# Value splits held back in the opening, four more products in the first expert's routing, token numbers as one sum: clustered attention and two expert layers on one core

## The reference, cut to what matters

```python
# attention, B=2, H=8, S=768, D=64, 16 clusters per head
q_assign = argmax(q_n @ c_n.T); k_assign = argmax(k_n @ c_n.T)     # normalised rows
scores = where(q_assign == k_assign, q @ k.T / 8, -1e9)
x = softmax(scores) @ v                                            # 1536 rows of 512
# first expert layer: 8 experts, each takes exactly 192 of the 1536 rows
for idx in argsort(-(x @ w_gate).flatten()):                       # the largest logit first
    tok, e = idx // 8, idx % 8
    if assigned[tok] >= 0 or counts[e] >= 192: continue
    assigned[tok] = e; counts[e] += 1
out[assigned == e] = relu(x[assigned == e] @ w1[e]) @ w2[e]        # 512 -> 1024 -> 512
# second layer: 4 experts, all rows through each, weighted by p
p = domain_probs / (domain_probs.sum(-1) + 1e-9)
out += p[:, e] * (relu(x @ w1[e]) @ w2[e])
```

## Time and profile before

| | |
|---|---|
| runs | 1019.85, 1019.0, 1020.62 us (median 1019.85) |
| profiled execution | 1019.42 us, span of its instructions 1017.6 us |
| mean granted TensorE clock | 0.995 |
| busy share of the span | TensorE 98%, VectorE 60%, ScalarE 44%, GpSimd 42% |
| opening, up to the first exponential | 20.4 us |
| routing with the first expert layer's products | about 297 to 515 us |

### The profile page before, as it was taken

The page is one execution under the profiler, slowest core; times in us unless marked ns, Lnnn a source line. Parts: engine busy times, 40 slices in busy tenths (PEclk is TensorE's granted clock), DMA queues, the critical chain, the costliest instruction groups (busy, mean ns, idle before and its releaser), DMA issues.

```text
span 1017.6 us, 18267 instructions
## 1 busy us (share of the span) xinstructions
PE 999.1 (98%) x6642; PEld 921.0 (91%) x6642; DVE 611.8 (60%) x1355; ACT 444.6 (44%) x862; POOL 425.4 (42%) x349
## 2 busy tenths in 40 slices
PE   8999999999999999999999999999999999999997
PEld 7889999999988999999999889999889998889995
DVE  6888888888867455556045445554486554455543
ACT  5888888888830111113342333322343323223320
POOL 5233233332201111112456757556567765566542
PEclk8999999999999999999999999999999999999999
DMA  5232323223155555556722122122112321221201
GB/s 159 56 78 67 86 73 85 77 81 82 31 126 182 183 182 181 182 182 205 249 75 83 42 83 72 53 84 67 57 63 83 125 83 45 80 83 51 74 1 63
DMA packets 87314, 99.63 MB, mean 98 GB/s; under 512 B 18097, under 2 KB 57041, under 8 KB 87249
## 3 DMA queue, kind: packets, MB, share of 16 engines
q1 hardware_dynamic: 84960, 92.38, 30.0%
q0 software_dynamic: 2288, 6.36, 1.9%
HBM read 79.81 MB, written 6.32 MB: 85 GB/s over the span
## 4 chain that ended last, share of the span: by engine, by line
PE 93%; DVE 3%; ACT 1%; POOL 1%; issue 1%; DMA 0%; DVEq 0%; POOLq 0%
PE ps_y L1569 10%; PE ps_y L1568 10%; PE ps_y L1567 10%; PE ps_h L1594 8%; PE ps_y L1609 8%; PE ps_h L1569 7%; PE ps_h L1567 7%; PE ps_h L1568 7%; PE ps_t L1448 6%; PE ps_s L1435 4%; PE ps_o L1462 3%; PE ps_o L1463 3%; PE ps_s L1436 3%; PE ps_m L1482 2%; PE ps_m L1409 2%; PE ps_m L1395 1%
## 5 line engine op out<-in xcount | busy, mean ns | idle before, releaser
L623 POOL TENSOR_TENSOR w_lo<-w_sum,w_hi 128x1792 fp32r<-128x1792 f32 x32 | 129.9, 4083 | 62.4 <-ACT w_hi L829 62.4
L1569 PE MATMUL ps_y<-b_lo,h_hi 128*128 128x512 f32 x384 | 149.7, 390 | 0.0
L1568 PE MATMUL ps_y<-b_hi,h_lo 128*128 128x512 f32 x384 | 149.7, 390 | 0.0
L1567 PE MATMUL ps_y<-b_hi,h_hi 128*128 128x512 f32 x384 | 149.4, 389 | 0.0
L1357 DVE SCALAR_TENSOR_TENSOR Y<-ps_y,ids_all,Y 128x512 f32<-128x512 f32 x84 | 63.0, 750 | 134.9 <-PE ps_y L1569 134.9
L1567 PE MATMUL ps_h<-x_hi,w_hi 128*128 128x384 f32 x384 | 128.6, 335 | 0.0
L1569 PE MATMUL ps_h<-x_lo,w_hi 128*128 128x384 f32 x384 | 128.5, 335 | 0.0
L1568 PE MATMUL ps_h<-x_hi,w_lo 128*128 128x384 f32 x384 | 128.4, 334 | 0.0
L629 POOL TENSOR_TENSOR b_lo<-b_raw,b_hi 128x2048 fp32r<-128x2048 f32 x16 | 74.0, 4622 | 116.2 <-ACT b_hi L836 115.4
L1008 DVE TENSOR_TENSOR p_lo<-ps_t,p_hi 128x384 fp32r<-128x384 f32 x192 | 99.9, 548 | 26.7 <-ACT p_hi L749 25.2
L999 DVE TENSOR_REDUCE neg_max<-ps_s 128x1 f32<-128x768 f32 x96 | 91.3, 951 | 14.8 <-PE ps_s L1436 14.3
(11 more groups left out here) (241 smaller groups left out, 2221.6 us busy)
## 6 DMA issues: line engine op xcount, KB each, us to landing
w_sum<-in_moe_w_dram SPq DMA_DIRECT2D x64, 256.0 KB, 3.2
b_raw<-in_moe_w_dram SPq DMA_DIRECT2D x16, 1024.0 KB, 5.2
raw_a<-in_moe_w_dram SPq DMA_DIRECT2D x8, 1024.0 KB
raw_b<-in_moe_w_dram SPq DMA_DIRECT2D x8, 1024.0 KB, 8.4
odd_a<-in_moe_w_dram SPq DMA_DIRECT2D x8, 1024.0 KB
odd_b<-in_moe_w_dram SPq DMA_DIRECT2D x8, 1024.0 KB, 8.3
khhT<-kqT SPq DMA_DIRECT2D x32, 192.0 KB, 3.1
raw_k<-in_k_dram SPq DMA_DIRECT2D x16, 192.0 KB, 2.4
```

The costliest lines, as they stand in the source:

```text
L623: g.tensor_tensor(w_lo[t][:], w_sum[t][:, 1:8], w_hi[t][:].bitcast(F32), ALU.subtract).then_inc(wlo_done[t], 1)
L1567: t_.matmul(dst, w_hi, x_hi, start=first, stop=False)
L1568: t_.matmul(dst, w_lo, x_hi, start=False, stop=False)
L1569: return t_.matmul(dst, w_hi, x_lo, start=False, stop=last)
```

## The change

- GpSimd waits for `one_ready >= 4`, the one-hots of the first two heads, before `split_first_values`. What follows on GpSimd is queued behind it.
- Eight more fillers (18 for 10) before the second head's cluster products.
- `F_FIRST` has two products for one behind the last three counts of phase 1, and six for five ahead of its ranks: four products more in phase 1, four fewer at the end of the list.
- The token number stands in three columns of `place` whose sum it is (4 times, 2 times, and the rest), and one reduction per number takes the place of copy and multiply-add. `place` is 15 columns wide and not 14.
- In phase 0 the closing of the chosen expert (three VectorE instructions) moves behind the first two token numbers.
- ScalarE copies `xe` in two halves, and TensorE's first product waits for the first half, the third for the second.

The places in the code that only shift columns are left out of the diff.

```diff
--- before.py
+++ after.py
@@ -52,7 +52,7 @@
     FAR = -(2.0 ** 100)
     BIG = 2.0 ** 125
 
-    F_FIRST = (0,) * 4 + (3, 1, 3, 1, 3, 1, 5, 0)
+    F_FIRST = (0,) * 4 + (3, 2, 3, 2, 3, 2, 6, 0)
     F_SECOND = (14, 2, 10, 2, 9, 2, 9, 2, 9, 2, 11, 0)
     F_PHASE = (12, 2, 7, 2, 6, 2, 6, 2, 6, 2, 9, 0)
     F_TOKENS = [0, 0, 8] + [8] * (E - 4)
...
@@ -96,8 +96,8 @@
         weigh = sb("weigh", [P, ND, P], BF16)
         first_e = sb("first_e", [P, E], F32)
         first_c = sb("first_c", [P, C], F32)
-        place = sb("place", [P, NT, 2 + 3 * E2], BF16)
-        place_f = sb("place_f", [P, NT, 2], F32)
+        place = sb("place", [P, NT, 3 + 3 * E2], BF16)
+        place_f = sb("place_f", [P, NT, 3], F32)
         rows = ExitStack()
         X = sb("X", [P, NT, H * (D + E)], F32, rows)
         rows.close()
...
@@ -199,7 +199,6 @@
         rank = sb("rank", [P, 2, NT], F32)
         slot = sb("slot", [P, 2, NT, 2], BF16)
         pen = sb("pen", [P, NT], F32)
-        place_lo = sb("place_lo", [P, 2], F32)
         ids = sb("ids", [P, E, 2, 1 + E2], I32)
         mix_lo = sb("mix_lo", [P, 2, E2], F32)
         mix_mid = sb("mix_mid", [P, 2, E2], F32)
...
@@ -501,11 +500,12 @@
                    allow_small_or_imprecise_dtypes=True).then_inc(const_ready, 1)
             g.iota(first_c[:], [[-1, C]], base=C, channel_multiplier=0,
                    allow_small_or_imprecise_dtypes=True).then_inc(const_ready, 1)
-            for i, (pattern, mult) in enumerate((([[P, B], [0, TPB]], 1), ([[0, B], [1, TPB]], 0))):
+            for i, (pattern, mult) in enumerate((([[4 * P, B], [0, TPB]], 4), ([[2 * P, B], [0, TPB]], 2),
+                                                   ([[0, B], [1, TPB]], 0))):
                 g.iota(place_f[:, :, i], pattern, base=0, channel_multiplier=mult,
                        allow_small_or_imprecise_dtypes=True).then_inc(const_ready, 1)
-            pool.wait_ge(const_ready, 9)
-            g.tensor_copy(place[:, :, 0:2], place_f[:]).then_inc(const_ready, 1)
+            pool.wait_ge(const_ready, 10)
+            g.tensor_copy(place[:, :, 0:3], place_f[:]).then_inc(const_ready, 1)
 
             def search_constants():
 
...
@@ -583,6 +583,7 @@
             pool.wait_ge(rows_split, 2)
             split_second(0, k_rows, qkv[1])
             split_second(1, q_rows, qkv[0])
+            pool.wait_ge(one_ready, 4)
             split_first_values()
             split_second_values()
             split_head(1, 0)
...
@@ -861,7 +862,8 @@
 
             def rows_1(m):
                 act.wait_ge(xt_full, m + 1)
-                s.copy(xe[:].rearrange("p (a c) m -> p a c m", a=2), xe_ps).then_inc(xe_done, 1)
+                for a in range(2):
+                    s.copy(xe[:, 2 * a:2 * a + 2, :], xe_ps[:, a]).then_inc(xe_done, 1)
 
             def y_out(m, j):
                 act.wait_ge(y_full, 2 * m + j + 1)
...
@@ -944,7 +946,7 @@
             clink(v_.reciprocal(cen_s[:, 6:7], cen_s[:, 5:6]))
             v_.tensor_scalar(cen2[:], spread(cen[:], 1, [P, 2, D]), cen_s[:, 6:7], None,
                              ALU.mult).then_inc(cen_rows, 1)
-            dve.wait_ge(const_ready, 10)
+            dve.wait_ge(const_ready, 11)
             dve.wait_ge(zeros_done, 2)
             dve.wait_ge(cen_hi, 1)
             v_.tensor_tensor(cenT[:, :, 1, :], ps_o[:, 0:P].rearrange("p (h c) -> p h c", c=C),
...
@@ -1146,39 +1148,37 @@
                     v_.tensor_tensor(rows_hot[:, :, c0:c1, :], spread(steps_2[:, c0:c1, :], 1, hot),
                                      spread(slot[:, n % 2], 2, hot), ALU.is_equal).then_inc(hot_ready, 1)
 
-            W = 2 + 3 * E2
+            W = 3 + 3 * E2
 
             def token_ids(n):
 
                 HS = CAP // 2
                 dve.wait_ge(ids_full, n + 2)
                 at = ps_tok[0:HS, 0:2 * W].rearrange("p (s a) -> p s a", s=2)
-                link(v_.tensor_copy(place_lo[0:HS, :], at[:, :, 1]))
-                v_.scalar_tensor_tensor(out=ids[0:HS, n, :, 0], in0=at[:, :, 0], scalar=float(TPB),
-                                        in1=place_lo[0:HS, :], op0=ALU.mult, op1=ALU.add).then_inc(ids_ready, 1)
+                with nc.allow_low_precision(reason="whole numbers under 2 ** 24"):
+                    v_.tensor_reduce(ids[0:HS, n, :, 0], at[:, :, 0:3], AX.X, ALU.add).then_inc(ids_ready, 1)
 
             def first_token_ids(s):
 
                 HS = CAP // 2
                 dve.wait_ge(ids_full, s + 1)
                 at = (ps_tok, ps_tok_0)[s]
-                link(v_.tensor_copy(place_lo[0:HS, s:s + 1], at[0:HS, 1:2]))
-                v_.scalar_tensor_tensor(out=ids[0:HS, 0, s, 0:1], in0=at[0:HS, 0:1], scalar=float(TPB),
-                                        in1=place_lo[0:HS, s:s + 1], op0=ALU.mult, op1=ALU.add).then_inc(ids_ready, 1)
+                with nc.allow_low_precision(reason="whole numbers under 2 ** 24"):
+                    v_.tensor_reduce(ids[0:HS, 0, s, 0:1], at[0:HS, 0:3], AX.X, ALU.add).then_inc(ids_ready, 1)
 
             def first_token_mix():
 
                 HS = CAP // 2
                 for s in range(2):
-                    add(v_.tensor_copy(mix_lo[0:HS, s], (ps_tok, ps_tok_0)[s][0:HS, 2 + 2 * E2:W]))
+                    add(v_.tensor_copy(mix_lo[0:HS, s], (ps_tok, ps_tok_0)[s][0:HS, 3 + 2 * E2:W]))
                 dve.wait_ge(r_step, r_count[0])
                 for s in range(2):
                     add(v_.tensor_tensor(mix_mid[0:HS, s], mix_lo[0:HS, s],
-                                         (ps_tok, ps_tok_0)[s][0:HS, 2 + E2:2 + 2 * E2], ALU.add))
+                                         (ps_tok, ps_tok_0)[s][0:HS, 3 + E2:3 + 2 * E2], ALU.add))
                 dve.wait_ge(r_step, r_count[0])
                 for s in range(2):
                     mm = v_.tensor_tensor(ids[0:HS, 0, s, 1:].bitcast(F32), mix_mid[0:HS, s],
-                                          (ps_tok, ps_tok_0)[s][0:HS, 2:2 + E2], ALU.add)
+                                          (ps_tok, ps_tok_0)[s][0:HS, 3:3 + E2], ALU.add)
                     if s == 0:
                         add(mm)
                     else:
...
@@ -1256,16 +1256,22 @@
                                              op0=ALU.is_equal, op1=ALU.mult))
                 rank_slots(n)
 
+                def close_chosen():
+
+                    add(v_.tensor_scalar(closing[:], e_b[:], e_top[:], GONE, ALU.is_equal, ALU.mult))
+                    link(v_.tensor_tensor(e_sum[:], e_sum[:], e_top[:], ALU.add))
+                    link(v_.tensor_tensor(logit[:], logit[:], spread(closing[:], 1, shape), ALU.add))
+
                 v_.tensor_scalar(e_num[:, n:n + 1], e_top[:], -1.0, float(E), ALU.mult,
                                  ALU.add).then_inc(e_chosen, 1)
-                add(v_.tensor_scalar(closing[:], e_b[:], e_top[:], GONE, ALU.is_equal, ALU.mult))
-                link(v_.tensor_tensor(e_sum[:], e_sum[:], e_top[:], ALU.add))
-                link(v_.tensor_tensor(logit[:], logit[:], spread(closing[:], 1, shape), ALU.add))
+                if n > 0:
+                    close_chosen()
                 take_slots(n)
                 slots_hot(n)
                 if n == 0:
                     for s in range(2):
                         first_token_ids(s)
+                    close_chosen()
                 link(v_.tensor_scalar(pen[:], slot[:, n % 2, :, 0], 0.0, GONE, ALU.is_lt, ALU.mult))
                 link(v_.tensor_tensor(logit[:], logit[:], spread(pen[:], 2, shape), ALU.add))
 
...
@@ -1543,7 +1549,7 @@
             clusters(first)
             tr_rows(second, 1)
             tr_rows(second, 2)
-            keep_on(gap, 10)
+            keep_on(gap, 18)
             clusters(second)
             tr_own(first)
             keep_on(gap, 26)
...
@@ -1584,8 +1590,8 @@
                 wt = (raw_a, odd_a)[m % 2]
                 j, a = st // KD, st % KD
                 i, f = j // KF, j % KF
-                if st == 0:
-                    pe.wait_ge(xe_done, m + 1)
+                if st < KD and st % 2 == 0:
+                    pe.wait_ge(xe_done, 2 * m + st // 2 + 1)
                 if f == 0 and a == 0:
                     pe.wait_ge((a_in, odd_a_in)[m % 2][i], 16 * (m // 2 + 1))
                 if a == 0:
```

More of the change, by code:

```diff
@@ L1190, in token_mix @@
                 at = ps_tok[0:HS, 0:2 * W].rearrange("p (s a) -> p s a", s=2)
-                link(v_.tensor_copy(mix_lo[0:HS], at[:, :, 2 + 2 * E2:]))
-                link(v_.tensor_tensor(mix_mid[0:HS], mix_lo[0:HS], at[:, :, 2 + E2:2 + 2 * E2], ALU.add))
-                v_.tensor_tensor(ids[0:HS, n, :, 1:].bitcast(F32), mix_mid[0:HS], at[:, :, 2:2 + E2],
+                link(v_.tensor_copy(mix_lo[0:HS], at[:, :, 3 + 2 * E2:]))
+                link(v_.tensor_tensor(mix_mid[0:HS], mix_lo[0:HS], at[:, :, 3 + E2:3 + 2 * E2], ALU.add))
+                v_.tensor_tensor(ids[0:HS, n, :, 1:].bitcast(F32), mix_mid[0:HS], at[:, :, 3:3 + E2],
                                  ALU.add).then_inc(mix_ready, 1)
```

8 lines of the change are left out of this document (4 added, 4 removed).

## The result

| | before | after |
|---|---|---|
| median of 7 runs each, us | 1020.27 (1019.0 to 1021.59) | 1023.27 (1021.96 to 1026.4) |
| profiled execution, us | 1019.42 | 1021.96 |
| its span, us | 1017.6 | 1020.1 |
| mean granted clock of TensorE | 0.995 | 0.998 |

What follows compares the result with a forecast made beforehand. TensorE, busy 999.1 of 1017.6 us, was taken as the bound. Terms -2.2 + 0.2 + 0.65 - 1.33 + 5.75 = +3.1 us on 1019.42 give 1022.5, or 1022.9 us as median; range 1017.0 to 1025.0.

Steps and rivals of the forecast that it cites:

- The opening, -2.2: Up to the first exponential: held-back splits and added fillers keep TensorE's clock up and start the scores sooner, -2.2 us.
- rival 2: Opening: the change does not hold the clock, which falls in the thin cluster products; only -0.9, 1024.2 us; 18%.
- The first two maxima: Opening, VectorE reading PSUM beside the held-back GpSimd splits: no loss, taken as 0, upper bound +1.0 us.
- rival 3: SyncE's queue in the opening: second head's key parts land after 27.8 us and the scores wait; 1025 us; 5%.
- Ranks to the first gather, +0.2: Routing: numbers come 0.3 to 0.6 us earlier, but phase 1's search waits for the moved closing; +0.2 us.
- The products in phase 1, +0.65: Phase 1's last three counts: second products delay the digit's matmul by 0.16 us twice and 0.33 once; +0.65 us.
- The tail, -1.33: Behind the routing, where TensorE never waits: four products of 0.33 us leave the tail, -1.33 us.
- The gathers, +5.75: Gathers 2 to 6: TensorE arrives 1.33 to 1.94 us sooner after the ranks and must wait; +5.75 us in all.
- the landing: Gathers 2 to 5: landing gains only the copy's 0.15 us, while TensorE arrives 1.33 us sooner after the ranks.
- rival 1: Transposes of experts 2 to 6: the gathers are not waited for; 1017.2 us against the median; 22%.
- Rival 4: Behind the gathers: new waits take the clock down; one fall of 2.7 us makes 1025.6 us, each further 2.7; 5%.

Runs made afterwards that it cites:

- experiment 3: The kernel before with only the opening changed (value splits held back, 18 fillers for 10): 1017.78 us, 0.9984 of before.
- experiment 2: The kernel before with only the four more products in phase 1 (`F_FIRST` changed): 1026.16 us, 1.0065 of before.
- experiment 4: The changed kernel with four products fewer ahead of phase 2's first count (10 for 14): 1016.76 us, 0.9975 of before.
- experiment 6: The kernel before with only the eight more fillers (18 for 10), value splits not held back: 1019.33 us, 0.9991 of before.
- experiment 7: The changed kernel with VectorE's token number made earlier in its phase, for phases 2 to 6: 1023.1 us, 1.0027 of before.
- experiment 8: The kernel before with two more products in phase 1, not four: 1023.15 us, 1.003 of before.
- experiment 10: The changed kernel with the opening and `F_FIRST` of before, leaving token numbers, closing and xe's split copy: 1019.94 us, 1.0 of before.
- experiment 1: The changed kernel with the old `F_FIRST`, so without its four more products: 1017.89 us, 0.9986 of before.
- experiment 5: The kernel before with only the hold of the value splits, ten fillers kept: 1018.78 us, 0.9991 of before.
- experiment 9: Experiment 4's kernel with GpSimd's search constants moved behind the loop over the heads: 1015.65 us, 0.9955 of before.

## Why the prediction was right

**The opening, -2.2: right step by step between the two profiled executions.** Taking off the 0.52 us by which the profiled execution began later, the transposes start at 13.54 (13.6 forecast), ScalarE's copies end at 15.89 (16.05), the scores start at 16.03 (16.05) and the first exponential stands at 18.20 (18.2). The clock held, so rival 2 did not occur. The assignment inside the term was untested then: the fillers give most of it, the hold 0.54 us. The first two maxima beside GpSimd's splits take 1.89 us together and took 0.96 each before: nothing lost, which was taken as 0 with a bound of +1.0. SyncE's load of the third head stood at 18.46 with the 0.52 taken off (18.4 forecast), and TensorE did not wait for the second head's parts: rival 3 did not occur.

**What the times show of it** is less, 1.6 us (experiment 3) for 2.2; the interval, 0.7 to 2.5, reaches over both. The term was worked out from one trace, and the old opening was long in that one: 11.34 us, where the mean of four is 10.97. That the single pair gave the 2.2 forecast is in part luck; 1.8 is the better estimate for a median.

**Ranks to the first gather, +0.2: right,** +0.18 (1.56 - 1.38). **The products in phase 1, +0.65: right,** 1.38 - 0.78 = +0.60; the digit's matmul stands 0.74 us behind the two products' start (0.73 forecast). **The tail, -1.33,** goes with the waits: together +3.58.

**The gathers, +5.75: right in mechanism and place, 0.7 us too large.** Forecast were 0.8, 1.18, 0.8, 1.18 and 1.79 us; measured 0.56, 1.02, 1.21, 0.59 and 1.67, 5.05. The step that failed is the landing, which I held at a fixed distance behind the token product. Expert 3's transposes stand 7.27 us behind its token product (386.94 to 394.21), and in the earlier trace rows the weight load that waited stood 7.74 behind (387.08 to 394.82): the copy, 0.15 us, and 0.3 more. Experts 4 and 5 did not repeat the pattern of 2 and 3 either (1.21 and 0.59 came in the other order). The scatter lies behind GpSimd: its two instructions take 0.96 or 0.97 and 0.91 or 0.92 us at every one of the five gathers, but from the end of the second to the transposes it is 2.22, 2.72, 2.88, 2.27 and 3.30 us. I took one value for all. Why a transfer takes 2.2 us once and 2.9 the next time no run here tells.

**The sum.** Forecast +3.1, measured +3.6 (2.7 to 4.5). The opening was given about half a microsecond of gain too much against the times, and the gathers 0.7 us of loss too much against the trace. The two misses have opposite signs and nearly cancel in the sum, which is luck.

**Rivals.** The gathers were waited for, so rival 1 fell. Rival 4 did not occur in the profiled execution of the change, but did in experiment 2's, behind 2.11 us; its price was put at 2.7 us, and it was 1.4 there, like the fall near 51 us, whose stretch was 1.3 us longer. One of the change's seven timed runs, 1026.40 us, has a mean granted clock of 0.993 where the others have 0.996 to 0.999, so the clock was down longer in it; where, no trace shows.

## What to carry to other kernels

Work that is moved into a gap is not free when the queue is in order: ask of each fixed place behind it which transfer it waits for, and whether the instruction that starts that transfer moved along; here four products of 0.33 us cost 5 us, because in five phases they set the token product, and with it the gather, four products later in the list while the transposes kept their place; taking four out at the next place (experiment 4) turned the loss into a gain. Compare openings from an event inside them, not from the span's start, which shifted by half a microsecond between the two executions here, and over more than one execution: the old opening alone spread over 1.3 us. Where a clock at half stands in one window, look for idle time ahead of it, and then for the same idle time elsewhere.

## What was not expected of the hardware

**The clock falls in some executions and not in others, behind the same wait.** Eleven profiled executions have the wait of 1.66 to 1.69 us near 50 us. In seven the granted clock is then 0.50 for about 3 us (experiments 2, 3, 4, 6, 7, 8 and 10), in four it stays at 1.00 (before, after, experiments 1 and 5). Where it fell, the stretch from the fourth head's transposes to the next cluster products is 7.80 us (50.10 to 57.90 in experiment 3), and 6.52 where it did not (50.38 to 56.90 in experiment 1): 1.3 us. The third and fourth rows are those where it fell:

```profile
50.38 0.54 PE L1401 MATMUL ps_m<-ident_r,k_rows 128*128 128x128 f32 x4 [1.66 <-POOL k_rows L544]
51.52 0.82 PE L1454 MATMUL ps_t<-ident,probs 128*128 128x128 f32 x6
...
50.10 0.53 PE L1396 MATMUL ps_m<-ident_r,k_rows 128*128 128x128 f32 x4 [1.66 <-POOL k_rows L544]
51.53 1.48 PE L1449 MATMUL ps_t<-ident,probs 128*128 128x128 f32 x6
```

Whether the fall is more frequent where the opening had none stays open: four of six traces with the new fillers show it, and three of five without. TensorE: Matmul & The Clock Gate, section "Part 1: The HAM clock gate", of the Trainium skill says that the gate's looking is not lined up with the start of the kernel; by it the same wait may fall well or ill from one execution to the next, and eleven traces agree with that, though none shows the alignment itself. In the one trace without the wait (experiment 9) the fall is not there.

**Of VectorE and GpSimd, the one that starts second waits for the rest of the other's operation.** In experiment 7 GpSimd's gather instruction starts at 390.07, inside VectorE's comparison of 128 x 1536 bfloat16 with two inputs in SBUF, of which 0.82 us are left (389.93 + 0.96), and takes 1.65 us for 0.97: 0.68 more. In experiment 1 it meets a float32 sum of 128 x 768 in the same way at expert 7, with 0.83 us left, and takes 0.69 more:

```profile
469.32 0.96 DVE L1302 TENSOR_TENSOR x_sum<-xs,x_sum 128x768 f32<-128x768 f32 x1
...
469.45 1.66 POOL L645 DMA_INDIRECT rows_in<-x_rows,ids  x1 [3.87 <-PE ps_h L1584]
```

Where 0.14 us are left, as in the changed kernel at expert 3 (389.31), it loses nothing. The same holds the other way round: in experiment 8 VectorE's comparison, 0.36 us in the second head, starts with 0.72 us left of GpSimd's split and takes 0.94, 0.58 more:

```profile
11.18 1.00 POOL L562 TENSOR_TENSOR v_rows<-raw_v,v_rows 128x384 fp32r<-128x384 f32 x1
...
11.46 0.94 DVE L982 TENSOR_TENSOR hit_c<-cl,best_c 128x192 f32<-128x192 f32 x1
```

So the loss is what is left of the other's operation less about 0.14 us, worked out from these rows. It fits the multiply of the earlier trace rows too: it starts at 12.24 inside a split that ends at 12.90, 0.66 us later, and is 0.51 us longer. That it is the inputs in SBUF and not another part of the operations was not tried. SBUF — State Buffer, section "Who interferes with whom", of the Trainium skill infers that an operation on two tensors does not hold up the work by which GpSimd issues DMAs. For the gather instruction the 1.65 and 1.66 us rows speak against that, and the measurement decides; which part of the instruction waits they don't show.

**Eight fillers of 0.06 us** decide over the clock for the next 3 to 7 us: with ten, the clock fell in all five traces, behind 0.33 us of idle and the thin products; with eighteen it stayed at 1.00 in all seven, through the same thin products, and 0.42 us of idle behind them did no harm (experiment 6). The eighteen also fill the 0.33 us of idle, so these runs don't tell whether it is the work or the missing gap that holds the clock.
